# A delta-rule attention stage on one core: the preparation of later groups placed between the steps of a group

## The reference

```python
for t in range(S):                      # q, k, v: 4 batches x 8 heads x 768 tokens x 48
    kt, vt, bt = (k_n[:, :, t], v[:, :, t], beta[:, :, t, None])      # k_n: k over its norm
    y[:, :, t] = np.einsum('bhd,bhde->bhe', q[:, :, t], state)
    v_old = np.einsum('bhde,bhd->bhe', state, kt)
    state = state + bt[:, :, :, None] * np.einsum('bhd,bhe->bhde', kt, vt - v_old)
...
x = attn_out.transpose(0, 2, 1, 3).reshape(B * S, H * D)       # 3072 tokens x 384
x = _moe_ref(x)      # gate, 8 Sinkhorn rounds, 8 experts 384 -> 1024 -> 384
return _moe2_ref(x)  # g = h * cos(h), 384 -> 2048 -> 384
```

## Time and profile before

| | us |
|---|---|
| median of 3 runs (2392.31 to 2399.72) | 2395.84 |
| profiled execution, its time | 2397.01 |
| profiled execution, its span in the trace | 2395.3 |
| PE busy / PEld busy in the span | 2229.8 / 1861.1 |
| DVE / ACT / POOL busy | 1002.8 / 745.5 / 699.9 |
| first instruction of the feed-forward part (ScalarE) | 381.58 |

### The profile page before, as it was taken

How to read it: one execution, slowest core, us unless ns; L and a number is a source line. 1 busy time by engine, 2 the same in 40 slices (tenths; PEclk the granted TensorE clock), 3 DMA queues, 4 the chain that set the end, 5 groups by cost and what they waited for, 6 DMA issues and landing times.

```text
span 2395.3 us, 39362 instructions
## 1 busy us (share of the span) xinstructions
PE 2229.8 (93%) x14696; PEld 1861.1 (78%) x14696; DVE 1002.8 (42%) x1583; ACT 745.5 (31%) x1262; POOL 699.9 (29%) x508
## 2 busy tenths in 40 slices
PE   4666685999999999999999999999999999999998
PEld 3666673888888888888888888888888887888887
DVE  5766542433223223233233233233232236777776
ACT  5555533111111111111111111111111125666665
POOL 2000001013233233233233233233233244444443
PEclk7666677999999999999999999999999999999999
DMA  4222111011111111110110111110111110000001
GB/s 120 68 69 68 55 43 40 1 42 26 44 31 27 31 29 41 31 31 26 44 31 26 31 33 37 31 31 26 44 31 26 31 34 6 27 13 14 0 14 66
DMA packets 68326, 84.82 MB, mean 35 GB/s; under 512 B 6096, under 2 KB 56976, under 8 KB 68240
## 3 DMA queue, kind: packets, MB, share of 16 engines
q1 hardware_dynamic: 68240, 83.59, 12.7%
HBM read 74.04 MB, written 4.82 MB: 33 GB/s over the span
## 4 chain that ended last, share of the span: by engine, by line
PE 66%; issue 11%; POOL 6%; POOLq 0%; DVE 0%; ACT 0%; DVEq 0%
PE yps L690 11%; PE hps L661 11%; PE yps L692 11%; PE yps L691 11%; PE hps L663 11%; PE hps L662 11%; POOL hlo L939 4%; POOL wlo L900 1%; PE hps L642 0%; PE hps L644 0%; PE hps L643 0%; POOLq L938 0%; DVE acc L1073 0%; POOL acc L922 0%; DVE xlo L956 0%
## 5 line engine op out<-in xcount | busy, mean ns | idle before, releaser
L1014 DVE SCALAR_TENSOR_TENSOR hlo<-hps,hhi 128x512 fp32r<-128x512 f32 x384 | 265.6, 692 | 934.5 <-ACT hhi L824 934.5
L824 ACT ACTIVATE hhi<-hps 128x512 fp32r<-128x512 f32 x384 | 229.8, 599 | 1278.0 <-PE hps L663 1278.0
L661 PE MATMUL hps<-xhi,whi 128*128 (+1 forms) x1440 | 562.0, 390 | 2.8 <-DVE scr L1099 2.4
L663 PE MATMUL hps<-xhi,wlo 128*128 (+1 forms) x1440 | 560.8, 389 | 0.0
L662 PE MATMUL hps<-xlo,whi 128*128 (+1 forms) x1440 | 560.8, 389 | 0.0
L922 POOL TENSOR_TENSOR acc<-acc,py 128x512 f32 x252 | 325.7, 1320 | 764.3 <-DVE py L1035 764.3
L690 PE MATMUL yps<-hhi,whi 128*128 128x512 f32 x1152 | 449.4, 390 | 7.7 <-issue 7.7
L691 PE MATMUL yps<-hlo,whi 128*128 128x512 f32 x1152 | 448.9, 390 | 0.0
L692 PE MATMUL yps<-hhi,wlo 128*128 128x512 f32 x1152 | 448.8, 390 | 0.0
L661 PEld LDWEIGHTS hps<-xhi,whi 128*128 128x128 f32 x1440 | 270.5, 188 | 61.1 <-issue 3.2
L663 PEld LDWEIGHTS hps<-xhi,wlo 128*128 128x128 f32 x1440 | 270.5, 188 | 56.2
(11 more groups left out here) (118 smaller groups left out, 1769.1 us busy)
## 6 DMA issues: line engine op xcount, KB each, us to landing
stage<-wcat SPq DMA_DIRECT2D x40, 768.0 KB, 4.3
pb<-p_scratch SPq DMA_DIRECT2D x90, 256.0 KB, 4.7
kqT<-kqt SPq DMA_DIRECT2D x48, 192.0 KB, 3.6
kb<-krow SPq DMA_DIRECT2D x6, 768.0 KB, 4.9
v<-vrow SPq DMA_DIRECT2D x6, 768.0 KB, 8.0
out<-acc SPq DMA_DIRECT2D x6, 768.0 KB, 3.8
acc<-yT SPq DMA_DIRECT2D x72, 48.0 KB, 2.0
acc<-yT SPq DMA_DIRECT2D x24, 32.0 KB, 1.9
```

Source lines behind the costliest of these rows:

```text
L661: pe.matmul(hps[bank][:, 0:TILE], w1(whi, buf, d, j), x_h, start=(d == 0), stop=False)
L663: mm = pe.matmul(hps[bank][:, 0:TILE], w1(wlo, buf, d, j), x_h, start=False, stop=(d == DC - 1))
L824: act.activation(hhi[:, j, :], hps[j % 2][:, 0:TILE], ACT.Relu).then_inc(s["hhi_done"], 1)
L1014: dve.scalar_tensor_tensor(out=hlo[:, j, :], in0=hps[j % 2][:, 0:TILE], scalar=0.0, in1=hhi[:, j, :].bitcast(F32), op0=ALU.max, op1=ALU.su ...
```

## The change

The products of keys with keys are taken apart from those of keys with queries. `key_products(g, r)` makes 64 columns for each of 8 pairs, with a transposed copy of the keys that is loaded by itself (`kta`), `keyed` takes them out. They share two PSUM banks with the merges. `query_products(i)` makes the query products of one step, and VectorE takes them out with the mask in one instruction (`masked`), one step ahead. Beta over the squared norm is no longer multiplied onto the keys: VectorE multiplies it onto W as it takes W out of PSUM (`updates`), which ScalarE did before. `keys` and `masking` are gone; the rows of the keys are loaded twice (`kn` for the norms, squared in place, and `kb` for the state).

In group g, steps 0 and 1 hold the four `key_products(g + 2)`, steps 2 and 3 the four merges of g + 1 with two quarters of the scatter each; step 2 the extract of g + 2. The leaf of g + 1 has its columns 13 to 30 in steps 0 and 1; columns 1 to 12 of g + 2 lie in steps 2 and 3. The first and the last column take one instruction instead of two. SyncE's loads and moves follow this order.

```diff
-LEAF_PARTS = ((1, 7), (7, 13), (13, 19), (19, 25), (25, 31))
-
...
+CHAINED = 2 * (L - 4) + 5
+RU = U // 4
+COLS = {0: ((13, 16), (16, 23)), 1: ((23, 27), (27, L - 1)), 2: ((), (1, 5)), 3: ((5, 7), (7, 13))}
...
+                sp.wait_ge(s["y_evac"], g * STEPS)
+                move_y(g - 1, 0)
+            for c in range(STEPS):
+                if g + 1 < NG:
+
+                    sp.wait_ge(s["w_done"], g * STEPS + c + 1)
+                    load_kq((g + 1) * STEPS + c)
+                if c < 2 and g + 3 < NG:
+                    load_kT(g + 3, c)
+                if c == 0 and g > 0:
+                    move_y(g - 1, 1)
+                if c == 2 and g + 4 < NG:
+                    load_k(g + 4)
...
+        def key_products(g, r):
+            if r % 2 == 0:
...
+            for j in range(RU):
+                for b in range(2):
+                    k = kT[b * CT:b * CT + HD, r * RU + j, :]
+                    mm = pe.matmul(rows(am_ps[r % 2], b)[:, j * CT:(j + 1) * CT], k, k, start=True, stop=True)
+            mm.then_inc(s["a_done"], 1)
...
+            if early:
+                key_products(g + 2, 2 * c)
...
             pe.wait_ge(s["m_evac"], 4 * g + 4)
-            pe.wait_ge(s["sc_done"], g + 1)
...
+            query_products(i + 1)
+            if late:
+                merge(g + 1, 2 * (c - 2))
             pe.wait_ge(s["w_evac"], i + 1)
...
+            if early:
+                key_products(g + 2, 2 * c + 1)
+            if late:
+                merge(g + 1, 2 * (c - 2) + 1)
...
+        def keyed(g, r):
...
+            act.wait_ge(s["a_done"], 4 * g + r + 1)
+            for j in range(RU):
+                n = r * RU + j
+                out = act.activation(A_[:, g % 2, n, :], am_ps[r % 2][:, j * CT:(j + 1) * CT], ACT.Copy, scale=bp[:, g, n:n + 1])
+            out.then_inc(s["a_evac"], 1)
...
+                act.activation(diag[L * q:L * q + L, :, :], A_[L * q:L * q + L, g % 2, :, o:o + L],
+                               ACT.Copy, scale=-1.0).then_inc(s["ext_done"], 1)
...
+                early = c < 2 and g + 2 < NG
+                late = c >= 2 and g + 1 < NG
+                if early:
+                    keyed(g + 2, 2 * c)
+                if c == 2 and g + 2 < NG:
+                    extract(g + 2)
+                if late:
+                    merged(g + 1, 2 * (c - 2))
+                state(g, c)
+                outputs(g, c)
+                if early:
+                    keyed(g + 2, 2 * c + 1)
+                if late:
+                    scatter(g + 1, 2 * (c - 2), 2 * (c - 2) + 2)
+                    merged(g + 1, 2 * (c - 2) + 1)
+                if c == 0 and g + 3 < NG:
+                    squares(g + 3)
...
+        def updates(g, c):
+            i = g * STEPS + c
+            dve.wait_ge(s["w_done"], i + 1)
+            if i > 0:
+
+                dve.wait_ge(s["y_done"], i)
+            dve.tensor_tensor(W[:, :, :], w_ps[:, 0:HEADS * HD].rearrange("p (n d) -> p n d", d=HD),
+                              bp[:, g, c * HEADS:(c + 1) * HEADS].unsqueeze(2).broadcast_to([P, HEADS, HD]),
+                              ALU.mult).then_inc(s["w_evac"], 1)
+
+        def masked(i):
+            if i >= NG * STEPS:
+                return
+
+            dve.wait_ge(s["p_done"], i + 1)
+            dve.tensor_tensor(P_[:, i % 2, :, :], p_ps[:, :].rearrange("p (n i) -> p n i", i=CT),
+                              mask[:, :].unsqueeze(1).broadcast_to([P, HEADS, CT]), ALU.mult).then_inc(s["p_evac"], 1)
 
...
         leaf_end(0)
-        masking(0)
-        keys(1)
+        normalise(2)
+        dve.wait_ge(s["mask_cut"], 2)
+        masked(0)
+        leaf_start(1)
+        leaf_init()
+        leaf(1, 13)
         for g in range(NG):
-            more = g + 1 < NG
-            if more:
-                leaf_start(g + 1)
-                leaf(*LEAF_PARTS[0])
+            near, far = g + 1 < NG, g + 2 < NG
             for c in range(STEPS):
                 residual(g, c)
-                if c == 1 and g + 2 < NG:
-                    sums(g + 2)
-                if c == 2 and g + 2 < NG:
-                    normalise(g + 2)
-                    keys(g + 2)
-                if more:
-                    leaf(*LEAF_PARTS[c + 1])
-            if more:
-                leaf_end(g + 1)
-                values(g + 1)
-                masking(g + 1)
+                if c < 2 and near:
+                    leaf(*COLS[c][0])
+                if c == 2 and far:
+                    leaf_start(g + 2)
+                if c == 3 and far:
+                    leaf(*COLS[c][0])
+                updates(g, c)
+                masked(g * STEPS + c + 1)
+                if c < 2 and near:
+                    leaf(*COLS[c][1])
+                    if c == 1:
+                        leaf_end(g + 1)
+                if c == 2:
+                    if g + 3 < NG:
+                        sums(g + 3)
+                    if far:
+                        leaf_init()
+                        leaf(*COLS[c][1])
+                if c == 3:
+                    if near:
+                        values(g + 1)
+                    if g + 3 < NG:
+                        normalise(g + 3)
+                    if far:
+                        leaf(*COLS[c][1])
```

More of the change, by code:

```diff
@@ L140, in load_v @@
-        def load_v(g):
-            sp.dma_start(v[:, g % 2, :, :].rearrange("p n d -> p (n d)"), vrow[g]).then_inc(s[f"v_loaded{g % 2}"], 16)
[L143 to L153, removed]
+            if g > 0:
+                sp.wait_ge(s["ss_done"], g)
@@ L155, in _ @@
         load_k(0)
-        for c in range(STEPS):
-            load_kq(0, c)
+        sp.dma_start(beta[:, :, :].rearrange("p g n -> p (g n)"), brow).then_inc(s["beta_loaded"], 16)
+        for part in range(2):
+            load_kT(0, part)
         load_k(1)
[L159 to L162, removed]
+        load_kT(1, 0)
+        load_kq(0)
+        load_rows(0)
+        load_kT(1, 1)
+        for i in range(1, STEPS):
+            load_kq(i)
@@ L163, in _ @@
+        load_k(2)
+        load_rows(1)
+        for part in range(2):
+            load_kT(2, part)
+        load_k(3)
         sp.dma_start(wgs[:, :, :], wgate).then_inc(gate_loaded, 16)
@@ L185, in _ @@
             sp.dma_start(stage[:, c], wcat[0, :, c]).then_inc(w_loaded[part], 16)
-        move_y(NG - 1)
+        sp.wait_ge(s["y_evac"], NG * STEPS)
+        for b in range(2):
+            move_y(NG - 1, b)
         for p in range(2):
@@ L191, in _ @@
     def _(pe):
[L192 to L205, removed]
@@ L276, in _ @@
         for g in range(2):
-            for c in range(STEPS):
-                prep(g, c)
-        merges(0)
+            for r in range(4):
+                key_products(g, r)
+        query_products(0)
+        for m in range(4):
+            merge(0, m)
         for g in range(NG):
-            ahead = g + 2 < NG
             for c in range(STEPS):
                 step(g, c)
-                if ahead and c > 0:
-                    prep(g + 2, c - 1)
-            if ahead:
-                prep(g + 2, STEPS - 1)
-            if g + 1 < NG:
-                merges(g + 1)
     @block.scalar
@@ new lines, in merged @@
+        def merged(g, m):
+            stg, k = divmod(m, 2)
+            n = slice(k * 16, (k + 1) * 16)
+            act.wait_ge(s["m_done"], 4 * g + m + 1)
+            if stg == 0:
+                out = act.activation(Y1[:, n, :], am_ps[k][:, :].rearrange("p (n i) -> p n i", i=L), ACT.Copy)
+            else:
+                for b in range(2):
+                    lo = b * CT
+                    out = act.activation(X[lo:lo + L, g % 2, n, L:2 * L], am_ps[k][lo:lo + L, :]
+                                         .rearrange("p (n i) -> p n i", i=L), ACT.Copy, scale=-1.0)
+            out.then_inc(s["m_evac"], 1)
@@ L348, in step, with state @@
+        def state(g, c):
             if not is_last(g, c):
@@ L360, in _ @@
         for g in range(2):
-            for c in range(STEPS):
-                prepared(g, c)
-            extract(g)
-        scatter(0)
-        merged(0)
-        for g in range(NG):
-            ahead = g + 2 < NG
-            for c in range(STEPS):
-                step(g, c)
-                if ahead and c == 0:
-                    squares(g + 2)
-                if ahead and c > 0:
-                    prepared(g + 2, c - 1)
-            if ahead:
-                prepared(g + 2, STEPS - 1)
-                extract(g + 2)
-            if g + 1 < NG:
-                scatter(g + 1)
-                merged(g + 1)
+            for r in range(4):
+                keyed(g, r)
+            extract(g)
+        squares(2)
+        scatter(0, 0, 4)
+        for m in range(4):
+            merged(0, m)
+        for g in range(NG):
+            for c in range(STEPS):
+                early = c < 2 and g + 2 < NG
+                late = c >= 2 and g + 1 < NG
+                if early:
[13 more added lines that the diff above has]
```

(1 more changed line is left out.)

280 lines of the change are left out of this document (148 added, 132 removed).

## The result

The changed kernel takes 2360.67 us (median of 4 runs, 2357.39 to 2365.89) against 2397.78 of before in the same comparison (2392.31 to 2402.35): a ratio of 0.985, 95% interval 0.982 to 0.988, 37 us less. The prediction said 2332, range 2318 to 2353. The direction was right, the size was not: the sum forecast 63.4 us less. The profiled execution took 2360.97, its span 2359.2; the feed-forward part begins at 346.20 instead of 381.58 and takes 2013.0 instead of 2013.7, so all but 0.7 of the difference lies in the attention.

The account below looks back on a forecast made before the run. VectorE was to be the fullest engine: 38.9 us of work plus a 2.9 stall, 41.8 a full group against 57.5. Saving 68.6, less 5.2 for the clock, gave 63.4 and a median of 2332 us, range 2318 to 2353.

Parts of the forecast that it names:

- the sum: Attention, all groups added up: first W of group 5 at 278.5 us, 68.6 saved, 63.4 after 5.2 for the clock.
- R of step 1 to R of step 2: VectorE's queue in step 1 of a full group: R, leaf columns, W, mask and the ending transposes take 9.4 us.
- the extract's stall: Step 2: VectorE's leaf start stands between R and W and waits for ScalarE's extract, 2.9 us (2.2 to 3.3) a group.
- one such fall: PE's clock falls in step 1 of every second of four groups: 1.3 us a group, 5.2 in all.
- Rival 3: PE's clock falls in most steps of the attention, adding 6.2 us a group: 2357 us, chance 22%.
- 1.84 just covers the 1.8: Step 3: VectorE's R and leaf columns, 1.84 us, hide the 1.8 after R until `w` is done, so W does not wait.
- covered by the 2.65: Step 0: leaf columns 13 to 15, 2.65 us on VectorE, hide the 1.8 after R until `w` is done.
- this costs nothing: Group boundary: ScalarE's last scatter half and `merged` delay `w` by 0.7 us, hidden by 2.65 of leaf columns before W.
- the 0.7 that the prediction named: Group boundary: delay of the next group's `w` by ScalarE's last `merged`, a cost only if the leaf-column cover were gone.
- The prediction's parts for group 4: Group 4: steps 0 and 1 take 19.7 us, then PE and ScalarE pace about 9 and 12.9; W to W 38.4.
- 0.5 was allowed: Steps after the first W of group 5: a query pass and a mask more, 0.2 us each, 0.5 taken off the saving.
- the ring: Repeating chain of one step, W, state product, S, `ks`, R, `w`, next W: 5.3 us if nothing else interferes.

Follow-up runs that it names:

- e2: Changed kernel with VectorE's transpose that starts the next leaf and waits for the extract moved from in front of W to behind the sums in step 2; 2345.2 us.
- e9: Changed kernel with constant filler products on PE, 4 before the wait for R in steps 1 and 2, 8 before the wait for W in step 2; 2347.5 us.
- e8: e6 with 4 constant filler products on PE in front of the wait for R in steps 1 and 2; 2329.0 us.
- e1: Changed kernel with 4 constant filler products on PE before the waits for R (steps 1 to 3) and for W (steps 0 and 1); 2359.8 us.
- e5: Changed kernel with 2 of the 16 pairs of products in every merge piece, the rest left out; 2341.1 us.
- e7: e2 with W taken out of PSUM by ScalarE before the extract instead of by VectorE, beta over the squared norm left out; 2355.9 us.
- e6: e2 with the second half of the scatter moved from step 3 to step 2, behind the evacuation of the second merge piece; 2336.7 us.

## Why the prediction missed

**Right.** In steps 0 and 1 the bound moved to VectorE's queue, and its durations were right to a few hundredths: from start to next start `updates` took 0.48 for 0.5 and `masked` 0.60 for 0.65, the eight evacuations took 1.75 to 1.80 for 1.8, R of step 1 to R of step 2 9.34 for 9.4, the extract's stall 2.98 to 3.00 for 2.9 in groups 0 to 2 (4.4 in group 3). e2 took that stall away and a group became 3.0 shorter. The first W was at 75.45 for 74.5. SyncE's order cost nothing to be seen.

**Wrong, the clock.** The step was "I take one such fall in every second of the four groups, so 1.3 a group and 5.2 in all". In the changed trace the clock fell in step 2 of each of groups 0 to 3, in step 1 of group 3, in group 4, and where groups 3, 4 and 5 begin; single stretches stayed low for 7 to 31 us, 44% of the four groups' time by the granted clock of 0.78. e9, which holds the clock by fillers and changes nothing else, gives 13 us back in the whole time where 5.2 was counted, 9 of them in the first four groups, and what its own fillers cost is already taken off.

Rival 3 (the clock falls in most steps, 2357 at 22%) had the condition that came, and a larger share would have been due to it: the earlier trace rows had shown one fall in two waits of 2.38, and the sum itself put several gaps of up to 2 us in each group. That its number lies only 4 us from the result is in part luck. It put the whole 6.2 us a group on the clock; e9 finds 2.3 there, and its groups are still 3.3 longer than those of the sum (44.7 for 41.4 in the mean of four).

**Wrong, the covers.** They were counted with `w` at the high clock, and there they held: in e8 W comes 1.85 after R in step 3 and 3.11 at the start of group 2, both without a wait, as "1.84 just covers the 1.8" and "covered by the 2.65" said. At the low clock a pass of `w` delivers 2.0 after its start instead of 1.2: in step 3 of groups 0 to 2 of the changed kernel W waited 1.58 and R 0.9 to 1.6. So this belongs to the clock, in a place where the sum had no term for it. The mask had no term at either clock. It needs the query pass behind `w`, and waits 0.3 to 0.4 more after W at the high clock and 0.9 to 1.2 at the low one; in e8 that is still 4.7 us in four groups, 1.2 a group.

**Wrong, the boundaries.** "this costs nothing" was said of ScalarE's last `merged`. Where groups 3, 4 and 5 begin, `w` waits 3.1, 2.1 and 2.0 us for it, and each time the next passes are slow:

```profile
261.36 1.94 PE L300 MATMUL w<-R,X 64*64 64x48 f32 x32 [2.07 <-ACT X L387]
```

W of group 4 comes 4.42 after R instead of 3.13. At the start of group 1 it came 3.83 after R, which looks like the 0.7 that the prediction named, but isn't: `w` was held to 120.44 by the last `merged`, and its pass was then broken by a pause of 0.91 without a releaser; without that pause the leaf columns would have covered it.

**Wrong, taken apart.** The terms were added as if independent. In e1 the gap of 1.89 at the stall undid the fillers, and in e2 removing the stall raised the clock from 0.76 to 0.87 as well. Group 4 shows it at the end: 44.2 in the changed kernel, 39.6 in e8, 38.4 predicted. (The prediction's parts for group 4, 10.3 + 9.4 + 9 + 12.9 less the 3.1 from R to W, give 38.5 up to `w` of group 5; W comes 1.2 behind `w`, so that its own sum is nearer to 39.7.) And the 278.96 of e8 for the first W of group 5 agrees with the 278.5 of the sum by chance: the sum has four stalls of 2.9 in it, e8 has none.

**Wrong, behind the sum.** The three steps from the first to the last W of group 5 took 21.5 us, before 17.2, where 0.5 was allowed. PE pauses there for 1.80 us without a releaser and runs slow passes behind it:

```profile
324.08 0.65 PE L316 MATMUL yps<-P_,W 64*48 64x64 f32 x16 [1.80 <-issue]
```

e8, which has no such pause there, took 16.5; e2 with one of 1.95 took 21.8. No experiment isolates this, but differences of a few microseconds between two single traces can lie in it.

**Open.** How long the low clock lasts: 7 to 31 us of nearly unbroken work in steps 2 and 3, some 7 us at the start of group 5. e5 says that it isn't the number of merge products. Whether they have a part in it is open: in e9 the clock fell in step 3 of groups 1 to 3, each time behind the second merge piece of step 2 and without a pause of PE. The 3.3 us a group that remain in e9 are explained by the waits in its trace, the mask's and those behind slow passes and pauses, and by the fillers' own cost; that is read from the trace, no run takes them away one by one. Why e7 is slower was settled only in part.

## What to carry to other kernels

When small matmuls of one chain are packed among others, price PE at both clocks and ask which gaps it will have; a stall on another engine that leaves PE idle can also cost the clock. A cover that just equals the time it must cover holds only while the covered engine keeps its fast clock: check it at the slow one too. Put nothing that waits for a third engine between two instructions of the ring (here the transpose in front of W). Where a gap is unavoidable, products of constants into a spare bank can pay: they did in the gaps (e9, e8), and did not when they were put where there was none while the gap at the stall stayed open (e1).

## Not expected of the hardware

PE ran at its low clock while busy without a break for 26 us (changed kernel, 145.65 to 172), and in e5 for 20 us with one pause of 1.55. The clock also fell without a pause in front: in e9 a pass took 1.61 at 149.60 and the next 1.89, though PE had not paused since 139.06. Filler products of 128 x 128 raised the granted clock from 0.76 to 0.93 (e9 against the changed kernel) and from 0.82 to 0.97 (e8 against e6); four took 1.16 us at the high clock and 2.07 at the low one. And PE sometimes waited for nothing that the profile shows, up to 2.7 us in the middle of a step, as in e9:

```profile
118.52 0.62 PE L231 MATMUL am<-kT 48*64 48x64 f32 x14 [2.74 <-issue]
```

Before had one such row of 1.3 us in this part; the changed kernel has 3.1 us in three rows, e8 some 5.8. In seven of the twelve traces of the changed kernel and its edits one stands in step 0 of group 1, at or just ahead of `w`. Their cause was not tested.
